# Local attention followed by two mixers on one core: score tables shared between head pairs, and two additions of the spatial product moved

## The chip, the cores and the metric

One core of a Trainium2 chip runs the whole program in one launch. The metric is device time in microseconds (us) of one execution. The kernel before was run three times; the median is 497.57 us. The engines are named as in the profile: PE (TensorE, the matrix engine), ACT (ScalarE), DVE (VectorE), POOL (GpSimd) and SP (which issues most transfers).

## What is computed

The input is an attention problem with batch 2, 8 heads, 768 positions and head size 64, all in fp32. For each head

    scores = q @ k.T / 8 + bias, with bias = -2**-(h+1) * distance
    (masked outside 8 global keys and a window of 96 keys back)
    x = softmax(scores) @ v

The slope of head h is 2^-(h+1) for h = 0 to 7. The heads' outputs are laid side by side to 512 features. Then follow two blocks: `u = x + (x mixed over positions by U V)`, `y = u + relu(u w1) w2`; and a gated block `h = relu(y w_in)`, split into u and v halves; v is normalised over features, multiplied by a 768 by 768 spatial matrix, a bias row is added, the result is multiplied by u and by `w_out`.

## The kernel before, in words

**Precision.** Most products run on PE as three passes of rounded operands: each fp32 operand is held as a rounded part (HI) and the rest (LO), and HI·HI, HI·LO and LO·HI are summed. A rounding is a copy on ACT or POOL, a rest is a subtraction on DVE or POOL.

**Attention.** The positions form 12 tiles t of 128 (six for each batch). Each tile is done in two steps of four heads, so there are 24 steps g, with t = g // 2 and hq = g % 2 the half of the heads. A step has two chunks, m = 0 and 1, and a chunk c = 2·hq + m holds two heads, 2c and 2c+1, on 64 partitions each. Each tile of 128 queries meets 256 keys (one block of 128 in the first tile of a batch); from the third tile on, the first 32 positions stand in place of the first 32 of the 256 keys, for the global keys.

- SP loads `qk_raw` (queries and keys of a tile, transposed; L372, three buffers) and `v_all` (L380). The first half of tile 0 is loaded from ACT's queue (L1126).
- `split_qk(g)` on POOL (L468 to 481): waits for the load, copies four 128x128 blocks to the HI part (a CAST of 128x512, L479) and subtracts for the LO part (a TENSOR_TENSOR of 128x512, L481). Steps 0 and 1 are split elsewhere, so that the first product starts soon: HI on ACT (L1133), LO on DVE (L719).
- `copy_k(g)` and `copy_v(g)` on POOL (L491, L501) put the 32 global positions into the key and value blocks. POOL's program, after a branch on the inputs (`windowed`, two register loads L304 and L305 and some ALU instructions), is splits 2 to 5 and then for each g: `copy_v(g)`, `copy_k(g+3)`, `split_qk(g+4)`, with some work for later stages in between (`round_V` L505 in iteration 4, `split_V` L513 in iterations 5 and 6, `split_early` L528 and `split_u` L536 from iteration 16 on).
- PE does in each loop step s: `turn(s)` (transposes of the probabilities, L1508), `turn_o(s-1)` and `turn_x(s-2)` (L1540, L1548), `scores(s+2)` (L1493), `weigh(s)` (probabilities by values, L1526). `scores(g)` waits for `qk_lo` of split g and, from the third tile of a batch on, for `copy_k(g)`; `weigh(g)` for `copy_v(g)`.
- `score_bias(g)` on DVE (L725 to 740, the instruction is at L736) adds the bias table to the scores, scales by -1/8 and takes the row's minimum in one instruction for each head. `exps(g)` on ACT (L1153) makes the exponentials.
- The tables: `bias0[:, h, :]` (128x128 for each head, for the first tile of a batch; L1136) and `bias[:, h, :]` (128x256 for each head; L1141) are copies of one distance table, scaled by the head's slope, all made on ACT. The eight of the first kind stand before ACT's branch; the eight of the second are made in pairs, between the exponentials of the first steps. `score_bias` waits in steps 0 to 3 until the table of its second head is set.

**The channel block** (about 93 to 349 us) and the products of the gated block (to 414 us) are PE work with the splits on the other engines beside it.

**The spatial product.** It is made in four groups q (two feature blocks of a batch each) as seven products of halves, each nine matmuls of 128x384 (L1826), into four banks. DVE adds them up: `add_bias(q, 0, 1)` (L1066) takes product 1 with the bias row out of bank 0, `add_bank` (L1062) takes the others, `gate_block` (L1073) multiplies by u, `split_gate` (L1080) makes the LO part after ACT has rounded the gated block (L1398). PE's third product of a group goes into bank 0 again and so waits for `add_bias(q, 0, 1)`. Every addition counts the semaphore `g_dve` up by one, seven for each group, in the same order before and after. DVE's order in a group is an order written by hand, the loop `for q in range(4)` at L1096. POOL does `add_far(q)` (L635) and splits beside it.

Of the kernel before, what the change touches and what calls it, by code (L numbers as in the profile page):

```python
# [13 lines left out]
P = 128  # L14
# [12 lines left out]
def build(nc, qk, qT, kT, v, cfg, U, V, w_ch, w_in, w_spT, b_sp, w_out, x_dram, out):  # L27
# [24 lines left out]
    with ExitStack() as ctx:  # L52
        base = (nc.sbuf_base + 63) // 64 * 64

        def at(name, shape, dtype, offset):
            return nc.alloc_sbuf_tensor_at(name, shape, dtype, offset=base + offset)
# [10 lines left out]
        part = [at(f"part{r}", [P, CT], F32, SLOT * 10 + 2048 * r) for r in range(3)]  # L67

        qk_split = at("qk_split", [P, 2, KD, 2, S], F32R, SLOT * 3)
        bias = at("bias", [P, H, KC], F32, SLOT * 9)  # L70
        bias0 = at("bias0", [P, H, P], F32, SLOT * 10)
        v_all = at("v_all", [P, NT, DM], F32, SLOT * 12 + 4096)
        prob = [at(f"prob{r}", [P, 2, KC], F32, SLOT * 14 + 2048 * r) for r in range(4)]
        probT = [at(f"probT{r}", [P, 2 * KC], F32, SLOT * 15 + 2048 * r) for r in range(4)]
# [106 lines left out]
        def sem(name):  # L181
            return ctx.enter_context(nc.semaphore(name))
# [5 lines left out]
        bias_set, iotas, ident_set, V_split = sem("bias_set"), sem("iotas"), sem("ident_set"), sem("V_split")  # L188
        qk_in = [[sem(f"qk_in{r}_{hq}") for hq in range(2)] for r in range(3)]
        v_in = [sem(f"v_in{i}") for i in range(NT)]  # L190
        qk0_hi, qk0_lo, qk_hi, qk_lo = sem("qk0_hi"), sem("qk0_lo"), sem("qk_hi"), sem("qk_lo")
        k_glob, v_glob = sem("k_glob"), sem("v_glob")
        stage_in = [sem(f"stage_in{r}") for r in range(2)]
# [23 lines left out]
            sem("wide_" + n) for n in ("qkv_in", "tables", "scored", "best", "exp")]  # L217
        w_turned, w_probT, w_out_ps, w_o, w_store, w_back, w_heads = [
            sem("wide_" + n) for n in ("turned", "probT", "out_ps", "o", "store", "back", "heads")]

        def heads(g, m):

# [229 lines left out]
        def _(pool):  # L452
# [5 lines left out]
            def count(tile, first, step, mult):  # L458
# [5 lines left out]
            pool.wait_ge(counted, 2)  # L464
            nc.gpsimd.affine_select(out=rel[:], in_=rel[:], compare_op=ALU.is_ge, fill=MASKED, base=P,
                                    pattern=[[-1, KC]], channel_multiplier=1).then_inc(iotas, 1)
            def split_qk(g):
                t, hq = divmod(g, 2)  # L468
                c, cols = slice(2 * hq, 2 * hq + 2), slice(t % NT * P, t % NT * P + P)
                hi, lo = qk_split[:, HI, c, :, cols], qk_split[:, LO, c, :, cols]  # L470
                raw = qk_raw[t % 3][:, c, :, :]
                pool.wait_ge(qk_in[t % 3][hq], 16 * (t // 3 + 1))
                if t >= NT:

                    pool.wait_ge(scored, 2 * (t - 5) + hq + 1)
                if t == NT:

                    pool.wait_ge(k_glob, globs_before(g - 1))
                nc.gpsimd.tensor_copy(hi, raw).then_inc(qk_hi, 1)  # L479
                pool.wait_ge(qk_hi, g - 1)  # L480
                nc.gpsimd.tensor_tensor(lo, raw, hi.bitcast(F32), ALU.subtract).then_inc(qk_lo, 1)  # L481
# [147 lines left out]
            def add_far(q):  # L629
# [4 lines left out]
                    pool.wait_ge(gate_lo, 4 * q)  # L634
                nc.gpsimd.tensor_tensor(gpart[3][:], gpart[0][:], b_row[:, HT:S], ALU.add).then_inc(far_bias, 1)  # L635

            near = windowed(pool)
            with pool.If(near):
                for g in range(2, 6):
# [53 lines left out]
        def _(dve):  # L693
# [28 lines left out]
            def score_bias(g, half=None):  # L722
                t = g // 2
                w = P * blocks(t)
                dve.wait_ge(scored, g + 1)  # L725
                for m in range(2) if half is None else (half,):
                    r = (2 * g + m) % 4
                    if g < 2:
                        dve.wait_ge(bias0_set, heads(g, m)[1][1] + 1)
                    elif g < 4:  # L730
                        dve.wait_ge(bias_set, heads(g, m)[1][1] + 1)
                    if g >= 2:
                        dve.wait_ge(turned, 2 * (g - 2) + m + 1)
                    for e, h in enumerate(heads(g, m)[1]):
                        k = g % 2 * 4 + 2 * m + e
                        last = vec.tensor_tensor_reduce(  # L736
                            prob[r][:, e, 0:w], s_bank[2 * (g % 2) + e][:, m * KC:m * KC + w],
                            bias0[:, h, :] if w == P else bias[:, h, :],
                            -SCALE, 3.0e38, ALU.add, ALU.min, row_min[:, k:k + 1])
                    last.then_inc(biased, 1)  # L740

            def take_probT(g):
# [351 lines left out]
                split_v_sums(q)  # L1094
            sum_v(2)
            for q in range(4):  # L1096
                add_bias(q, 0, 1)
                add_bank(q, 0, 0, 1, 2, 1)
                add_bias(q, 2, 3)

                dve.wait_ge(g_act, by_act(item_no("s", 0)))
                gate_block(q, 0, 3)
                dve.wait_ge(far_bias, q + 1)
                add_bank(q, 1, 3, 2, 4, 0)
                split_gate(q, 0)
                add_bank(q, 1, 1, 3, 5, 4)
                gate_block(q, 1, 5)
                if q == 2:

                    sum_v(3)  # L1110
                add_bank(q, 2, 0, 2, 6, 2)
                gate_block(q, 2, 6)
                split_gate(q, 1)
                add_bank(q, 3, 3, 3, 7, 0)
                gate_block(q, 3, 7)
                split_gate(q, 2)
                split_gate(q, 3)
                if q == 2:
                    split_v_ones(3)
                    split_v_sums(3)  # L1120
# [3 lines left out]
        def _(act):  # L1124
# [4 lines left out]
            sc.activation(tiny[:, 0:1], ident[:, 0:1], ACT.Exp)  # L1129
            for hq in range(2):  # L1130
                c = slice(2 * hq, 2 * hq + 2)
                act.wait_ge(qk_in[0][hq], 16)
                sc.activation(qk_split[:, HI, c, :, 0:P], qk_raw[0][:, c, :, :], ACT.Copy).then_inc(qk0_hi, 1)  # L1133
            act.wait_ge(dist0_set, 1)
            for h in range(H):
                sc.activation(bias0[:, h, :], dist0[:], ACT.Copy, scale=-(2.0 ** -(h + 1)) / SCALE  # L1136
                              ).then_inc(bias0_set, 1)

            def set_bias(first):
                for h in range(first, first + 2):  # L1140
                    sc.activation(bias[:, h, :], dist[:], ACT.Copy, scale=-(2.0 ** -(h + 1)) / SCALE  # L1141
                                  ).then_inc(bias_set, 1)

            def exps(g, half=None):
                w = P * blocks(g // 2)
# [85 lines left out]
            with act.If(near):  # L1231
                for s in range(-2, QUADS):
                    if s >= 2:
                        take_probT(s)
                    if s == 13:
                        split_stage(0)
                        copy_z(0)
                    if 0 <= s + 1 < QUADS:
                        add_eps(s + 1)
                    if s == 14:  # L1240
                        round_z(0)
                    if s in (-2, 0, 1):
                        set_bias((0, None, 4, 6)[s + 2])
                    if s >= 2:
                        take_xT(s - 2, s)
                    if 0 <= s + 2 < QUADS:
                        exps(s + 2)
                    if s == -1:
                        set_bias(2)
                    if s == 19:  # L1250
                        split_stage(1)
                    if s in (16, 18, 20, 22):
                        round_u((s - 16) // 2)
# [657 lines left out]
```

## Time and profile before

| what | value |
|---|---|
| median of 3 runs | 497.57 us (497.57 to 500.12) |
| the profiled execution: time | 497.54 us |
| the profiled execution: span from first to last instruction | 495.7 us |
| PE busy | 488.5 us, 99% |
| DVE busy | 311.8 us, 63% |
| POOL busy | 248.9 us, 50% |
| ACT busy | 222.2 us, 45% |
| moved by DMA | 36.27 MB |

The time around the span is 497.54 - 495.7 = 1.8 us. In a timeline row stand the start in us from the span's start, the length in us, the engine, the line of the kernel, the operation, what it writes and reads, the shapes and a count; several instructions of one kind in a row are merged. The square brackets hold the idle time of the engine just before it and what ended it. A name with a q behind the engine (POOLq) is the engine's instruction queue.

### The profile page before, as it was taken

How to read it: one execution, taken by the hardware profiler on the slowest of the kernel's cores; microseconds unless marked ns; L12 is line 12 of the kernel's file. 1: busy time of each engine (PE TensorE's matmuls, PEld its weight loads, DVE VectorE, ACT ScalarE, POOL GpSimd, SP SyncE). 2: the span in 40 equal slices, each digit the busy share in tenths (PEclk: the TensorE clock that was granted, in tenths of full speed). 3: DMA queues.
4: the chain of work that ended last, by engine and by line, in shares of the span. 5: the costliest groups of instructions: out<-in, count | busy, mean ns of one | idle time of the engine just before them, and what ended most of it. 6: DMA issues, size and time to landing. Idle time of an engine off the chain costs nothing.

```text
span 495.7 us, 7920 instructions
## 1 busy us (share of the span) xinstructions
PE 488.5 (99%) x2786; PEld 407.7 (82%) x2786; DVE 311.8 (63%) x726; ACT 222.2 (45%) x521; POOL 248.9 (50%) x219
## 2 busy tenths in 40 slices
PE   8999999999999999999999999999999999999997
PEld 7788677887888888888888888888888889998985
DVE  5888788511279466465655555557868888878600
ACT  7988889532234633232342322405542265333121
POOL 5898576443336666854566636323884202930000
PEclk9999999999999999999999999999999999999999
DMA  8723501132222322012222020120113000001022
GB/s 239 266 91 107 194 2 44 46 127 86 80 85 91 128 85 84 21 65 86 85 87 85 1 85 21 66 63 2 63 65 116 2 0 2 0 1 44 22 89 102
DMA packets 14552, 36.27 MB, mean 73 GB/s; under 512 B 2480, under 2 KB 2480, under 8 KB 14512
## 3 DMA queue, kind: packets, MB, share of 16 engines
q1 hardware_dynamic: 12640, 32.35, 19.5%
q10 hardware_dynamic: 1872, 3.41, 1.8%
q8 instruction: 23, 0.38, 0.3%
q14 instruction: 17, 0.14, 0.1%
HBM read 32.61 MB, written 3.15 MB: 72 GB/s over the span
## 4 chain that ended last, share of the span: by engine, by line
PE 93%; ACT 3%; DVE 2%; DMA 1%; issue 0%; SPq 0%; ACTq 0%
PE bank L1744 15%; PE bank L1470 13%; PE bank L1676 9%; PE bank L1601 9%; PE bank L1773 9%; PE bank L1766 9%; PE bank L1826 7%; PE bank L1844 7%; PE bank L1526 4%; PE bank L1508 4%; PE bank L1493 3%; ACT prob L1153 1%; PE bank L1540 1%; PE bank L1548 1%; DMA qk_raw<-in_qk 1%; DVE gated_lo L1080 1%
## 5 line engine op out<-in xcount | busy, mean ns | idle before, releaser
L520 POOL TENSOR_TENSOR w_slot<-stage,w_slot 128x1024 fp32r<-128x1024 f32 x30 | 73.3, 2451 | 64.8 <-ACT w_slot L1223 64.8
L918 DVE TENSOR_TENSOR uT<-bank,uT 128x512 f32<-128x512 f32 x68 | 45.8, 689 | 25.4 <-PE bank L1773 23.3
L1153 ACT ACTIVATE prob<-prob,row_min 128x256 f32<-128x256 f32 (+1 forms) x96 | 45.9, 480 | 7.4 <-DVE row_min L736 7.4
L1744 PE MATMUL bank<-u_op,s_slot 128*128 128x512 f32 x192 | 47.6, 389 | 0.0
L1676 PE MATMUL bank<-hid,w_slot 128*128 128x512 f32 x192 | 46.9, 393 | 0.0
L1601 PE MATMUL bank<-u_split,w_slot 128*128 128x512 f32 x192 | 46.5, 391 | 0.0
L1766 PE MATMUL bank<-hid,w_slot 128*128 128x512 f32 x192 | 46.1, 389 | 0.0
L1773 PE MATMUL bank<-hid,w_slot 128*128 128x512 f32 x192 | 46.1, 389 | 0.0
L956 DVE TENSOR_TENSOR part<-part,bank 128x512 f32<-128x512 f32 x40 | 27.4, 686 | 26.2 <-PE bank L1744 25.8
L1676 PEld LDWEIGHTS bank<-hid,w_slot 128*128 128x128 f32 x192 | 35.7, 188 | 8.2 <-issue 0.9
L1766 PEld LDWEIGHTS bank<-hid,w_slot 128*128 128x128 f32 x192 | 36.0, 188 | 7.5
L1773 PEld LDWEIGHTS bank<-hid,w_slot 128*128 128x128 f32 x192 | 36.0, 188 | 7.5
L1744 PEld LDWEIGHTS bank<-u_op,s_slot 128*128 128x128 f32 x192 | 36.0, 188 | 7.5
L1601 PEld LDWEIGHTS bank<-u_split,w_slot 128*128 128x128 f32 x192 | 35.7, 188 | 7.5 <-issue 0.2
L1223 ACT ACTIVATE w_slot<-stage 128x1024 fp32r<-128x1024 f32 x32 | 33.2, 1051 | 12.7 <-DMA stage<-in_w_ch 12.7
L736 DVE CUSTOM_DVE_ANT_0 prob<-bank,bias 128x256 f32<-128x256 f32 (+1 forms) x96 | 32.9, 398 | 7.0 <-PE bank L1493 5.5
L1744 PE MATMUL bank<-u_op,w_slot 128*128 128x512 f32 x144 | 36.5, 389 | 0.0
L928 DVE SCALAR_TENSOR_TENSOR hid<-bank,hid 128x512 fp32r<-128x512 f32 x16 | 11.1, 691 | 39.5 <-ACT hid L1276 39.3
L567 POOL TENSOR_TENSOR s_slot<-s_raw,s_slot 128x1024 fp32r<-128x1024 f32 x8 | 19.2, 2401 | 32.6 <-ACT s_slot L1228 32.6
L1844 PE MATMUL bank<-in_slot,y_split 128*128 128x512 f32 x144 | 32.8, 389 | 0.0
L1470 PE MATMUL bank<-y_split,in_slot 128*128 128x512 f32 x144 | 32.8, 389 | 0.0
L1470 PEld LDWEIGHTS bank<-y_split,in_slot 128*128 128x128 f32 x144 | 27.0, 188 | 5.6
(149 smaller groups left out, 958.7 us busy)
## 6 DMA issues: line engine op xcount, KB each, us to landing
stage<-in_w_ch SPq DMA_DIRECT2D x32, 512.0 KB, 3.3
qk_raw<-in_qk SPq DMA_DIRECT2D x23, 256.0 KB, 4.5
v_all<-in_v SPq DMA_DIRECT2D x12, 256.0 KB, 4.9
out_dram<-o_stage ACTq DMA_DIRECT2D x12, 256.0 KB, 2.0
stage<-in_w_spT SPq DMA_DIRECT2D x6, 384.0 KB, 3.1
stage<-in_w_in SPq DMA_DIRECT2D x4, 512.0 KB, 4.3
stage<-in_w_out SPq DMA_DIRECT2D x2, 512.0 KB, 3.9
V_raw<-in_V SPq DMA_DIRECT2D x4, 96.0 KB, 4.4
```

The costliest lines, as they stand in the source:

```text
L520: nc.gpsimd.tensor_tensor(dst[:, LO, :], stage[n % 2][:, 0:w], dst[:, HI, :].bitcast(F32), ALU.subtract).then_inc(w_lo, 1)
L918: vec.tensor_tensor(y, y_bank(e)[:], y, ALU.add).then_inc(y_sum, 1)
L1153: last = sc.activation(prob[r][:, e, 0:w], prob[r][:, e, 0:w], ACT.Exp, bias=row_min[:, k:k + 1], scale=-1.0, accum_out=row_sum[:, q:q + 1])
L1223: sc.activation(dst[:, HI, :], stage[n % 2][:, 0:w], ACT.Copy).then_inc(w_hi, 1)
L1470: last = mm(out_ap, lhs(a), rhs(c), start=(n == 0), stop=(n == 3 * len(terms) - 1))
L1601: last = mm(h_bank[f % 2][:], w_slot[f][:, a, k * P:(k + 1) * P], u_split[:, m, k, :], start=(k == 0 and p == 0), stop=(k == KD - 1 and p ...
L1676: last = mm(c_bank[k][:], w_slot[f][:, a, 512 + k * P:512 + (k + 1) * P], hid[f % 2][:, m, :], start=(f == 0 and a == HI and m == HI), sto ...
L1744: last = mm(seven_bank[held][:], lhs, u_op[op][:, m, k, :], start=not more and k == 0 and p == 0, stop=k == 1 and p == 2, skip_group_check ...
L1766: mm(y_bank(e + k)[:], w[r][:, a, 512 + k * P:512 + (k + 1) * P], hid2[r][n][:, m, :], start=(a == HI and m == HI), stop=False, skip_group ...
L1773: last = mm(y_bank(e + k)[:], w[r][:, a, 512 + k * P:512 + (k + 1) * P], hid2[r][n][:, m, :], start=False, stop=(a == LO), skip_group_chec ...
L1826: last = mm(s_banks(q)[held][:, 0:HT], lhs, sp_op[j][:, m, SP_AT[op], :], start=not more and j == 0 and n == 0, stop=j == TC - 1 and n == ...
L1844: last = mm(dst[:], y_split[c][:, a, k, r * P:(r + 1) * P], in_slot[k][:, m, FH:2 * FH], start=(k == 0 and p == 0), stop=(k == KD - 1 and ...
```

## The change

1. The queries of the second chunk (m = 1) of every step are multiplied by four in place before they are split: one POOL instruction `tensor_scalar` over 128x128 for each of the 24 steps (`spread_q`). For the heads of the second chunk, slope and score are both a quarter of what the first chunk's tables fit, so the scores taken four times and the first chunk's table are added, and the result is scaled by -1/32 instead of -1/8. Four tables of each kind are left (heads 0, 1, 4, 5), and ACT makes the four wide ones before the first exponentials.
2. `spread_q(0)` and `spread_q(1)` stand before POOL's branch; ACT's HI copies of tile 0 wait for them. In `split_qk` the CAST waits for the spread of its own step.
3. In the spatial product, `add_bias(1, 0, 1)` and `add_bias(2, 0, 1)` stand before `split_gate(q, 3)` of the group before them instead of behind it.

```diff
-        bias = at("bias", [P, H, KC], F32, SLOT * 9)
-        bias0 = at("bias0", [P, H, P], F32, SLOT * 10)
+        bias = at("bias", [P, 4, KC], F32, SLOT * 9)
+        bias0 = at("bias0", [P, 4, P], F32, SLOT * 10)
...
+            def spread_q(g):
+                t, hq = divmod(g, 2)
+                queries = qk_raw[t % 3][:, 2 * hq + 1, Q, :]
+                pool.wait_ge(qk_in[t % 3][hq], 16 * (t // 3 + 1))
+                nc.gpsimd.tensor_scalar(queries, queries, SPREAD, None, ALU.mult).then_inc(q_spread, 1)
+
             def split_qk(g):
...
-                pool.wait_ge(qk_in[t % 3][hq], 16 * (t // 3 + 1))
+                spread_q(g)
...
+                pool.wait_ge(q_spread, g + 1)
                 nc.gpsimd.tensor_copy(hi, raw).then_inc(qk_hi, 1)
...
+            for g in range(2):
+                spread_q(g)
             near = windowed(pool)
...
                     if g < 2:
-                        dve.wait_ge(bias0_set, heads(g, m)[1][1] + 1)
+                        dve.wait_ge(bias0_set, 2 * g + 2)
                     elif g < 4:
-                        dve.wait_ge(bias_set, heads(g, m)[1][1] + 1)
+                        dve.wait_ge(bias_set, 2 * (g - 2) + 2)
...
-                            bias0[:, h, :] if w == P else bias[:, h, :],
-                            -SCALE, 3.0e38, ALU.add, ALU.min, row_min[:, k:k + 1])
+                            (bias0 if w == P else bias)[:, 2 * (g % 2) + e, :],
+                            -SCALE / SPREAD if m else -SCALE, 3.0e38, ALU.add, ALU.min, row_min[:, k:k + 1])
...
             for q in range(4):
-                add_bias(q, 0, 1)
+                if q in (0, 3):
+                    add_bias(q, 0, 1)
...
                 split_gate(q, 2)
+                if q < 2:
+
+                    add_bias(q + 1, 0, 1)
                 split_gate(q, 3)
...
-                act.wait_ge(qk_in[0][hq], 16)
+                act.wait_ge(q_spread, hq + 1)
...
-            for h in range(H):
-                sc.activation(bias0[:, h, :], dist0[:], ACT.Copy, scale=-(2.0 ** -(h + 1)) / SCALE
-                              ).then_inc(bias0_set, 1)
...
+            for n, slope in enumerate(SLOPES):
+                sc.activation(bias0[:, n, :], dist0[:], ACT.Copy, scale=-slope / SCALE).then_inc(bias0_set, 1)
...
-                    if s in (-2, 0, 1):
-                        set_bias((0, None, 4, 6)[s + 2])
+                    if s == -2:
+                        set_bias(0)
...
-                    if s == -1:
-                        set_bias(2)
+                    if s == -2:
+                        set_bias(1)
```

## Rows read from the trace of the kernel before

**Rows 1.** The page: PE's busy time, POOL in 40 slices, the chain's shares

```profile
PE 488.5 (99%) x2786; PEld 407.7 (82%) x2786; DVE 311.8 (63%) x726; ACT 222.2 (45%) x521; POOL 248.9 (50%) x219
...
POOL 5898576443336666854566636323884202930000
...
PE 93%; ACT 3%; DVE 2%; DMA 1%; issue 0%; SPq 0%; ACTq 0%
```

**Rows 2.** Timeline of the first 22 us: ACT and DVE at the start

```profile
5.53 0.63 ACT L1133 ACTIVATE qk_split<-qk_raw 128x512 fp32r<-128x512 f32 x1 [0.55 <-DMA qk_raw<-in_qk]
...
15.21 0.71 ACT L1141 ACTIVATE bias<-dist 128x256 f32<-128x256 f32 x2
...
16.05 0.42 DVE L736 CUSTOM_DVE_ANT_0 prob<-bank,bias 128x256 f32<-128x256 f32 x1 [0.67 <-issue]
```

**Rows 3.** Timeline of PE, 9 to 50 us: scores(4), turn(3), weigh(7)

```profile
16.14 0.98 PE L1493 MATMUL bank<-qk_split 64*128 64x256 f32 x12
...
19.07 1.09 PE L1508 MATMUL bank<-ident,prob 128*128 128x128 f32 x8
...
35.28 1.09 PE L1526 MATMUL bank<-probT,v_all 128*64 128x128 f32 x16
```

**Rows 4.** Timeline of POOL, 0 to 95 us

```profile
6.29 1.14 POOL L479 CAST qk_split<-qk_raw 128x512 fp32r<-128x512 f32 x1 [3.84 <-DMA qk_raw<-in_qk]
7.51 1.28 POOL L481 TENSOR_TENSOR qk_split<-qk_raw,qk_split 128x512 fp32r<-128x512 f32 x1
...
14.48 0.53 POOL L491 CAST qk_split<-qk_split 128x128 fp32r<-128x128 f32 x2
...
17.19 0.29 POOL L491 CAST qk_split<-qk_split 128x128 fp32r<-128x128 f32 x1 [0.26 <-PE bank L1493]
...
21.58 0.29 POOL L491 CAST qk_split<-qk_split 128x128 fp32r<-128x128 f32 x1 [1.85 <-PE bank L1493]
...
24.50 0.39 POOL L501 COPY v_all<-v_all 32x256 f32<-32x256 f32 x1
25.04 0.29 POOL L491 CAST qk_split<-qk_split 128x128 fp32r<-128x128 f32 x1
...
33.86 0.39 POOL L501 COPY v_all<-v_all 32x256 f32<-32x256 f32 x1
34.20 0.28 POOL L491 CAST qk_split<-qk_split 128x128 fp32r<-128x128 f32 x1
```

**Rows 5.** Lines L304 and L638, POOL's first register load and its branch: ns min/median/max, first and last start

```profile
L304 POOLq TENSOR_LOAD <-cfg_i x1: 518/518/518, 4.0 to 4.0; - x1
...
L638 POOLq COMPARE_BRANCH  x2: 38/39/40, 5.2 to 91.1; - x2
```

**Rows 6.** POOL's groups by line and form: busy us, mean ns | idle us before

```profile
L491 POOL CAST qk_split<-qk_split 128x128 fp32r<-128x128 f32 x16 | 4.5, 288 | 9.8 <-PE bank L1493 9.6
...
L453 POOL MEMSET ident<- 128x128 f32 x1 | 0.2, 204 | 0.3 <-POOLq L1901 0.3
```

**Rows 7.** Lines L626, L479 and L1073: ns min/median/max, first and last start

```profile
L626 POOL TENSOR_TENSOR v_one<-v_far,v_one x9: 450/770/786, 423.5 to 428.7; 128x128 fp32r<-128x128 f32 x9
...
L479 POOL CAST qk_split<-qk_raw x22: 603/609/1142, 6.3 to 76.9; 128x512 fp32r<-128x512 f32 x22
...
L1073 DVE TENSOR_TENSOR gpart<-gpart,gate_u x16: 557/558/1389, 419.5 to 468.6; 128x384 f32<-128x384 f32 x16
```

**Rows 8.** Timeline of all engines, 410 to 441 us: the ends of groups 0 and 1

```profile
426.89 1.55 DVE L1080 TENSOR_TENSOR gated_lo<-gpart,gated_hi 128x384 fp32r<-128x384 f32 x2
...
428.36 0.54 DVE L1066 TENSOR_TENSOR gpart<-bank,b_row 128x384 f32<-128x384 f32 x1
428.96 1.83 PE L1826 MATMUL bank<-sp_op,v_one 128*128 128x384 f32 x9 [0.81 <-DVE gpart L1066]
...
439.66 0.56 DVE L1080 TENSOR_TENSOR gated_lo<-gpart,gated_hi 128x384 fp32r<-128x384 f32 x1
...
440.74 1.86 PE L1826 MATMUL bank<-sp_op,v_one 128*128 128x384 f32 x9 [0.59 <-DVE gpart L1066]
```

More of the change, by code:

```diff
@@ L190, in build @@
         v_in = [sem(f"v_in{i}") for i in range(NT)]
+        q_spread = sem("q_spread")
         qk0_hi, qk0_lo, qk_hi, qk_lo = sem("qk0_hi"), sem("qk0_lo"), sem("qk_hi"), sem("qk_lo")
@@ L219, in build @@
             sem("wide_" + n) for n in ("turned", "probT", "out_ps", "o", "store", "back", "heads")]
+        SPREAD = 4.0
         def heads(g, m):
@@ L1131, in _, with set_bias @@
                 c = slice(2 * hq, 2 * hq + 2)
-                act.wait_ge(qk_in[0][hq], 16)
+                act.wait_ge(q_spread, hq + 1)
                 sc.activation(qk_split[:, HI, c, :, 0:P], qk_raw[0][:, c, :, :], ACT.Copy).then_inc(qk0_hi, 1)
             act.wait_ge(dist0_set, 1)
-            for h in range(H):
-                sc.activation(bias0[:, h, :], dist0[:], ACT.Copy, scale=-(2.0 ** -(h + 1)) / SCALE
-                              ).then_inc(bias0_set, 1)
[L1139 to L1142, printed above, removed]
+            SLOPES = [2.0 ** -(h + 1) for h in (0, 1, 4, 5)]
+            for n, slope in enumerate(SLOPES):
+                sc.activation(bias0[:, n, :], dist0[:], ACT.Copy, scale=-slope / SCALE).then_inc(bias0_set, 1)
+            def set_bias(hq):
+                for n in (2 * hq, 2 * hq + 1):
+                    sc.activation(bias[:, n, :], dist[:], ACT.Copy, scale=-SLOPES[n] / SCALE).then_inc(bias_set, 1)
             def exps(g, half=None):
```

## The prediction

> **What bounds the kernel now.** I read the page first: PE is busy 99% of the span and carries 93% of the chain that ended last [rows 1]. So a cut on ACT alone is worth nothing unless it lets PE go on sooner; what counts is where PE stands still. The page's second part says where another engine is full: POOL has 8 and 9 tenths in the first slices (12.4 us each) [rows 1]. Then I read the places that the change touches.
>
> At the start, DVE's addition of a bias in the second half of its fourth step begins at 16.05 us after 0.67 us idle; the tables that it needs are made on ACT from 15.21 to 15.92 us [rows 2]. That is a real wait for a table. From 19.07 us on, where `turn(3)` starts, PE runs without a gap up to the last of the steps [rows 3]. POOL waits 1.85 us for PE before 21.58 us, so it has caught up there; then it works with hardly a gap to `copy_v(7)`, which starts at 33.86 us, ends 34.25 us [rows 4], and is needed by `weigh(7)` at 35.28 us [rows 3]. That is a margin of only 1.0 us, and all that the change adds to attention goes onto POOL. In the spatial product PE stands 0.81 and 0.59 us before the third product of groups 1 and 2, both times for DVE's L1066 [rows 8].
>
> **Tables.** Removed are four of the 128x128 copies and four of the 128x256 copies on ACT (two of the latter take 0.71 us [rows 2], so 1.4 us in all). None of it counts by itself. What counts is DVE's wait of 0.67 us at 16.05 us, which goes away: its last table is now made before the first exponentials.
>
> **The spread at the start.** ACT's second HI copy began at 5.53 us, as its data landed [rows 2]. Now one POOL instruction of 128x128 stands between. The trace has no `tensor_scalar` on POOL. The nearest rows are the CAST of 128x128 with one input, 0.29 us, the MEMSET of 128x128 with none, 0.20 us [rows 6], and the TENSOR_TENSOR of 128x128 with two inputs, 0.45 us at least and 0.77 us at the median, much of it beside DVE's work [rows 7]. I take 0.29 us, because it also reads one input. To this comes the wait for its own end: from the end of the CAST at 7.43 us to the subtraction at 7.51 us it is 0.08 us [rows 4]. So the price p of one spread in POOL's row of work is 0.37 us, with 0.28 and 0.85 us as ends. ACT's copy, and all of the first steps behind it, come 0.35 to 0.4 us later. With 0.67 us saved later, this nets a gain of at most 0.3 us at `turn(3)`, if POOL keeps up.
>
> **POOL's row of work, step by step.** Its branch comes 1.24 us after its first register load begins (4.00 to 5.24 us [rows 5]). The loads now stand behind `spread_q(1)`, which can't start before 5.53 us; so the branch ends at about 5.55 + 1.24 = 6.79 us, and `spread_q(2)` starts, with 0.16 us allowed for its way to the engine, at about 6.95 us instead of the CAST at 6.29 us [rows 4], 0.66 us later. Each split adds p. So:
> - `copy_k(4)` (the first of the two at 14.48 us [rows 4]) has splits 2 to 5 ahead of it: it ends at 14.77 + 0.66 + 4p = 16.91 us. `scores(4)` waits for it and began at 16.14 us [rows 3]: now 16.97 us. That comes back in part, as PE then stood for the probabilities (from `scores(4)` to `turn(3)` it took 2.93 us, back to back it takes 1.92 us). `turn(3)` starts at 16.97 + 1.92 = 18.89 us, 0.2 us sooner than before.
> - Up to 21.58 us POOL loses 0.66 + 6p (splits 2 to 7) less the gaps of 0.26 and 1.85 us, and less about 0.05 us of overlap that was lost there: 6p - 1.50 = 0.72 us late. Splits 8, 9 and 10 add 3p; 0.20 us are won back at 25.04 us, where the way from the copy of the values to that of the keys took 0.54 us instead of the usual 0.34 us (33.86 to 34.20) [rows 4]. `copy_v(7)` ends at 34.25 + 9p - 1.70 = 35.88 us.
> - `weigh(7)` waits for it and starts at 35.94 us instead of 35.28 us [rows 3]: attention is 9p - 2.67 = 0.66 us slower from there on. Since PE runs without a gap afterwards, nothing gives that back.
>
> Behind that, the pressure falls: splits 11 to 14 bring p each, but the two V splits are over. POOL's last copies of a batch become 3 us late, and the first load of values of the second batch waits for them; I cost that at nothing, hidden by PE's steps 10 and 11, but it is the next thing to be late. The spreads from there to the end of attention I cost at nothing too: POOL is at 5 to 8 tenths there [rows 1], and PE's own steps cover them; without that cover each would cost up to p.
>
> **The lock between POOL and DVE.** The first CAST took 1.14 us, the median one 0.61 us, and DVE's gate product took 1.39 us beside POOL and 0.56 us alone [rows 7]. The first CAST ran beside DVE's two-input subtraction, which ends at 6.96 us. If the neighbour is what made it long, the CAST now starts at 7.32 us, when the subtraction (also 0.35 us later) is over, and takes 0.61 us, while the spread before it waits up to 0.36 us for it: POOL gains about 0.25 us. I kept the 1.14 us in the sum, as the same instruction's own row, and price the other as a rival. The Trainium skill ("SBUF — State Buffer", section "SBUF: two separate sides") says that a VectorE instruction with two SBUF inputs and a GpSimd instruction that reads SBUF shut each other out for their whole length; by it the sum would be the rival's.
>
> **The spatial additions.** Two `split_gate` take 1.55 us together from 426.89 us, and `add_bias` starts at 428.36 us; behind only one of them it starts at about 427.66 us, and PE goes on 0.06 us after its end, at 428.25 instead of 428.96 us: 0.7 us [rows 8]. PE's products before it end at 428.96 - 0.81 = 428.15 us, so 0.1 us of the wait is left. At the second place the last `split_gate` starts at 439.66 us, PE at 440.74 us [rows 8]. Group 1 is 0.7 us ahead, and DVE's row there hangs on PE's products, so `add_bias` can start at 439.66 - 0.70 = 438.96 us and PE at 439.57 us: 1.17 us ahead in all. `split_gate(q, 3)`, now later by 0.54 us, holds up nothing: what is queued behind it on DVE, the second bank's addition, starts with the old order's delay at the latest, and POOL's far bias, which waits for that one, comes no later than before. From 441 us PE has no gap, so the 1.17 us stay.
>
> **Sum.** 497.54 + 0.66 - 1.17 = 497.03 us, against the profiled execution's 497.54 us, which is 0.03 us from the median. I forecast 497.0 us.
>
> **Rivals.** 0.5% is 2.49 us, about what a measurement of this kernel tells from no change.
> - *The spread is cheap* (p = 0.28 us): then `copy_v(7)` ends at 35.07 us and attention is 0.15 us faster. Time: 497.54 - 0.15 - 1.17 = 496.2 us. For it: a MEMSET of the size takes 0.20 us. Against: it reads nothing. Chance 0.25.
> - *The first CAST gets short* and the rest is as forecast: POOL's row is 0.25 us sooner, 497.03 - 0.25 = 496.8 us. For it: 1.14 against 0.61 us [rows 7]. Against: a first use of an instruction may be long by itself. Chance 0.1.
> - *The spread is dear, and the kernel slower.* POOL's `tensor_scalar` may run like its two-input form. Place: `copy_v(7)` before `weigh(7)`. Attention costs 9p - 2.67, so the kernel is slower than before from 9p = 3.84, p = 0.43 us; with 0.53 us it is 498.5 us, with 0.85 us 501.3 us. It passes 0.5% only from p = 0.70 us. Chance 0.18, a third of it above that point.
> - *The moved additions bring nothing*, because PE then waits for the next addition of the group: 497.54 + 0.66 = 498.2 us. Against: the additions behind it keep their order and start sooner. Chance 0.07.
> - The forecast's own case: 0.4.
>
> **Numbers.** The range from 495.7 to 499.6 us takes in the cheap spread with its full start gain and the dear one up to p = 0.65 us. Faster by over 0.5% would need 495.05 us, beyond every case: 0.02. Slower by over 0.5%: 0.06 for the dear spread's upper third, and 0.01 for a late load of values, so 0.07. Same: 0.91.
>
> **What would show it.** In the changed trace: 24 POOL instructions of 128x128 at about 0.29 us; `copy_v(7)` ending near 35.9 us and PE idle before `weigh(7)` for 0.8 us with POOL's L501 line as releaser; PE idle before `scores(4)` behind POOL's key copy; no DVE wait of 0.67 us at the fourth step; PE's gaps before the third product at 0.3 us or less. The forecast is wrong if POOL's spread is not near 0.29 us, if PE meets no wait for POOL at 35 us, or if attention's last PE instruction does not lie 0.4 to 0.9 us later than before.

## The result, and the profile after

| | before | after |
|---|---|---|
| median of 6 runs | 497.71 us (497.57 to 500.12) | 499.89 us (499.42 to 501.13) |
| ratio after / before | | 1.0047, 95% interval 1.0031 to 1.0062 |
| profiled execution: time, span | 497.54, 495.7 us | 501.13, 499.3 us |
| forecast | | 497.0 us, range 495.7 to 499.6 us |

The kernel became 2.2 us slower, where I forecast 0.5 us faster. That is just within the 0.5% that I had called no change, but the interval leaves out 1, and the time lies outside the range. Of several kernels here, the one before too, some executions take 1 to 3 us longer than the rest; in the two of them that were profiled (of e3 and e8 below) PE works at half its pace up to about 13 us (24 products in 2.83 us instead of 1.56 us), and they are in all medians and ratios.

The page of the kernel after answers to [rows 1]: PE is busy 2.1 us longer although it does the same work, POOL 13.7 us longer, and POOL's second to fifth slices have 9, 9, 8 and 7 tenths where they had 8, 9, 8 and 5.

```profile
PE 490.6 (98%) x2786; PEld 410.3 (82%) x2786; DVE 310.5 (62%) x726; ACT 221.0 (44%) x513; POOL 262.6 (53%) x243
...
POOL 6998789444335687635576356231886201950000
...
PE 92%; POOL 6%; issue 1%; DMA 1%; POOLq 0%; ACT 0%; ACTq 0%
```

The last line holds the first warning: POOL, which had no share in the chain that ended last, now has 6% of it. The groups by line and form name what is new. The columns are busy us and mean ns, then the idle time before:

```profile
L491 POOL CAST qk_split<-qk_raw 128x512 fp32r<-128x512 f32 x22 | 13.5, 612 | 2.4 <-POOL qk_raw L476 0.3
L476 POOL TENSOR_SCALAR qk_raw<-qk_raw 128x128 f32<-128x128 f32 x24 | 13.3, 553 | 6.5 <-DMA qk_raw<-in_qk 4.8
...
L503 POOL CAST qk_split<-qk_split 128x128 fp32r<-128x128 f32 x16 | 4.6, 289 | 1.1 <-PE bank L1511 1.1
```

The spread takes 0.55 us in the mean, the CAST of the same size 0.289 us. That CAST was my model for it.

**The start.** In the timeline of ACT and DVE, the second HI copy comes at 5.96 us instead of 5.53 us [rows 2], as forecast, and DVE's first addition of a bias at 8.22 us instead of 7.80 us:

```profile
5.96 0.63 ACT L1151 ACTIVATE qk_split<-qk_raw 128x512 fp32r<-128x512 f32 x1 [0.56 <-POOL qk_raw L476]
...
8.22 0.29 DVE L750 CUSTOM_DVE_ANT_0 prob<-bank,bias 128x128 f32<-128x128 f32 x1 [0.90 <-ACT bias L1156]
```

**POOL's row of work** (its timeline from 0 to 95 us). From 6.70 us to 54 us it has no idle time left but two waits of 0.16 us and the short ways between its own instructions; the gaps of 0.26 and 1.85 us of [rows 4] are filled.

```profile
5.37 0.56 POOL L476 TENSOR_SCALAR qk_raw<-qk_raw 128x128 f32<-128x128 f32 x1 [0.63 <-DMA qk_raw<-in_qk]
6.70 1.00 POOL L476 TENSOR_SCALAR qk_raw<-qk_raw 128x128 f32<-128x128 f32 x1 [0.78 <-DMA qk_raw<-in_qk]
7.77 0.61 POOL L491 CAST qk_split<-qk_raw 128x512 fp32r<-128x512 f32 x1
8.47 1.28 POOL L493 TENSOR_TENSOR qk_split<-qk_raw,qk_split 128x512 fp32r<-128x512 f32 x1
9.83 0.53 POOL L476 TENSOR_SCALAR qk_raw<-qk_raw 128x128 f32<-128x128 f32 x1
10.43 0.61 POOL L491 CAST qk_split<-qk_raw 128x512 fp32r<-128x512 f32 x1
...
17.67 0.53 POOL L503 CAST qk_split<-qk_split 128x128 fp32r<-128x128 f32 x2
...
38.35 0.39 POOL L513 COPY v_all<-v_all 32x256 f32<-32x256 f32 x1
```

From one CAST to the next it is 10.43 - 7.77 = 2.66 us; before it was 1.90 us (8.74 to 10.64 us). So a spread costs 0.76 us in this row: 0.53 us of work, 0.07 us from its end to the CAST that waits for it, and 0.13 us because it starts 0.08 us after the end of the subtraction ahead of it, where the CAST used to start 0.05 us before that end (the three rounded parts give 0.73). `copy_v(7)` ends at 38.74 us.

**PE** (its timeline from 5 to 46 us) waits for POOL at three places: `scores(4)`, `weigh(6)` and `weigh(7)`.

```profile
18.10 0.97 PE L1511 MATMUL bank<-qk_split 64*128 64x256 f32 x12 [0.49 <-POOL qk_split L503]
...
20.03 1.09 PE L1526 MATMUL bank<-ident,prob 128*128 128x128 f32 x8
...
33.53 1.09 PE L1544 MATMUL bank<-probT,v_all 128*64 128x128 f32 x16 [0.62 <-issue]
...
38.79 1.90 PE L1544 MATMUL bank<-probT,v_all 128*64 128x128 f32 x16 [1.80 <-POOL v_all L513]
40.62 1.91 PE L1526 MATMUL bank<-ident,prob 128*128 128x128 f32 x8
...
43.80 1.09 PE L1544 MATMUL bank<-probT,v_all 128*64 128x128 f32 x16
```

Against [rows 3], `turn(3)` is 0.96 us late and `weigh(7)` 3.51 us. Then it gets worse: `weigh(7)` and the turn behind it take 1.90 and 1.91 us, where both kinds take 1.09 us elsewhere. The windows (PE busy with its count, granted clock, DMA share, GB/s) show why:

```profile
37.00:38.00 1.00, 0.00 (x0) 1.00 0.11 25
38.00:39.00 1.00, 0.21 (x4) 0.96 0.00 0
39.00:42.00 3.00, 3.00 (x23) 0.50 0.00 0
42.00:43.00 1.00, 1.00 (x9) 0.83 0.00 0
```

Behind the wait of 1.80 us PE was granted 0.50, which is 1.2 GHz, for some 3 us. `weigh(8)` starts at 43.80 us instead of 38.73 us, 5.07 us late, so the clock added 1.56 us. PE's first product of the channel block comes 5.09 us later (98.09 against 93.00 us in the chain), and the same lateness stands at the start of the spatial product (419.19 against 414.08 us).

**The spatial product** wins back more than forecast. In the timeline, PE has no wait before the third product of groups 1 and 2 [rows 8]:

```profile
432.80 0.55 DVE L1080 TENSOR_TENSOR gpart<-bank,b_row 128x384 f32<-128x384 f32 x1
433.40 1.85 PE L1844 MATMUL bank<-sp_op,v_one 128*128 128x384 f32 x9
...
443.72 0.55 DVE L1080 TENSOR_TENSOR gpart<-bank,b_row 128x384 f32<-128x384 f32 x1
444.45 1.72 PE L1844 MATMUL bank<-sp_op,v_one 128*128 128x384 f32 x9
```

In the chain that ended last the stretch is now one piece of PE:

```profile
419.19 33.23 PE bank L1844 x189
452.42 8.20 PE bank L1488 x36
```

Before, it took 34.75 us (414.08 to 448.83 us) for these products: 1.52 us less. Together: 497.54 + 5.09 - 1.52 = 501.11 us, against 501.13 us measured. Of the six executions after, two lie at 501.1 us and four at 499.4 to 500.1 us. A sum without the clock's 1.56 us gives 497.54 + 3.51 - 1.52 = 499.53 us, which is where the four lie. That this is the difference of the groups is likely, but the mean granted clock of each execution does not show it for this kernel: it is 0.993 and 0.997 in the two, 0.996 to 1.0 in the four, and the profiled execution has a second stretch at 0.50 near its start (from 9 to 11 us), which others may have too. e6 below shows it better.

### The profile page after: what moved, and what is told of

It is laid out like the page before. It is cut to its first block, busy times and chain, and to the rows that moved or that the text cites. A ratio compares the mean times of both kernels' runs of the same rounds, so it can differ in the third digit from the quotient of the medians.

```text
span 499.3 us, 7936 instructions
## 1 busy us (share of the span) xinstructions
PE 490.6 (98%) x2786; PEld 410.3 (82%) x2786; DVE 310.5 (62%) x726; ACT 221.0 (44%) x513; POOL 262.6 (53%) x243
## 4 chain that ended last, share of the span: by engine, by line
PE 92%; POOL 6%; issue 1%; DMA 1%; POOLq 0%; ACT 0%; ACTq 0%
PE bank L1762 15%; PE bank L1488 13%; PE bank L1844 9%; PE bank L1694 9%; PE bank L1619 9%; PE bank L1791 9%; PE bank L1784 9%; PE bank L1862 7%; PE bank L1544 4%; PE bank L1526 3%; PE bank L1511 3%; POOL qk_split L493 2%; POOL qk_raw L476 1%; POOL qk_split L491 1%; PE bank L1558 1%; PE bank L1566 1%
## 5 line engine op out<-in xcount | busy, mean ns | idle before, releaser
L1862 PEld LDWEIGHTS bank<-in_slot,y_split 128*128 128x128 f32 x144 | 27.0, 188 | 5.6
```

What stands on the lines that cost most here:

```text
L1862: last = mm(dst[:], y_split[c][:, a, k, r * P:(r + 1) * P], in_slot[k][:, m, FH:2 * FH], start=(k == 0 and p == 0), stop=(k == KD - 1 and ...
```

## The experiments

The theory was: the loss is POOL's load ahead of `copy_v(7)`, at twice the price that I gave a spread, and the moved additions are a gain by themselves. The rivals were: the later start (spreads 0 and 1, POOL's later branch) is what costs; the additions bring nothing; the loss comes from the tables or DVE. In the table, "attention" is the part of the loss that is not the moved additions: the median less e1's 496.02 us, and for e2 and e6, whose additions are not moved, less the 497.6 us of the kernel before.

| kernel | median us (runs) | ratio to before, 95% interval | attention |
|---|---|---|---|
| e1, additions alone | 496.02 (12) | 0.9972 (0.9955 to 0.9989) | 0 |
| e2, all but the additions | 501.44 (6) | 1.0077 (1.0057 to 1.0097) | +3.8 |
| e3, V splits late | 497.72 (12) | 1.0003 (0.9993 to 1.0013) | +1.7 |
| e4, spreads on ACT | 496.44 (11) | 0.9974 (0.9961 to 0.9988) | +0.4 |
| e5, spread twice | 510.17 (4) | 1.0250 (1.0226 to 1.0273) | +14.2 |
| e6, POOL load alone | 499.67 (8) | 1.0040 (1.0026 to 1.0055) | +2.1 |
| e7, first tiles plain | 499.65 (11) | 1.0045 (1.0032 to 1.0058) | +3.6 |
| e8, e7 with late spreads on ACT | 496.75 (12) | 0.9984 (0.9964 to 1.0004) | +0.7 |

### The two parts of the change, each alone

e1 is the kernel before with only the two additions moved; e2 is the kernel after with them put back.

```diff
             for q in range(4):
-                add_bias(q, 0, 1)
+                if q in (0, 3):
+                    add_bias(q, 0, 1)
...
                 split_gate(q, 2)
+                if q < 2:
+                    add_bias(q + 1, 0, 1)
                 split_gate(q, 3)
```

> The kernel before with only the two moved additions. Theory A (the moved additions take PE's two gaps away, and attention pays for it): PE's waits of 0.81 and 0.59 us behind add_bias are gone, the stretch of the three first spatial groups takes 33.2 us instead of 34.75 us, and the time is 1.5 us below the kernel before (about 496.1 us). Theory B (PE's gaps closed only because attention's delay had shifted the other engines): 0 to 0.5 us below.

> The changed kernel with the two additions put back. Theory A: attention ends 4 to 5 us late as in the changed kernel and nothing is won back, so the time is 1.5 us above the changed kernel: 501.2 to 501.6 us, 3.5 to 4 us above the kernel before. Theory B: as the changed kernel, 499.5 to 500.1 us.

e1 took 496.02 us, 1.6 us less than before. In its chain, 108 matmuls follow each other without DVE between them, from 428.25 to 447.28 us; before, the same stretch had a piece of DVE's work from 435.48 to 440.74 us and ended at 448.83 us.

```profile
427.72 0.48 DVE gpart L1066
428.20 0.04 issue
428.25 19.03 PE bank L1829 x108
447.27 8.20 PE bank L1473 x36
```

e2 took 501.44 us, 1.5 us more than the whole change. So the two parts add up, and the additions are worth 1.5 us in either kernel. The rest of the change costs 3.8 us.

### Is it POOL's load, or the start?

e6 is the kernel before with a multiplication by 1.0 of the same 128x128 block in each of the 22 splits on POOL, and nothing else: the tables, the first two steps and the values stay as they were.

```diff
+                queries = qk_raw[t % 3][:, 2 * hq + 1, Q, :]
+                nc.gpsimd.tensor_scalar(queries, queries, 1.0, None, ALU.mult).then_inc(q_spread, 1)
+                pool.wait_ge(q_spread, g - 1)
                 nc.gpsimd.tensor_copy(hi, raw).then_inc(qk_hi, 1)
```

> The kernel before, with all its tables and nothing in front of POOL's branch, and one POOL multiplication by 1.0 of 128x128 in each split from step 2 on (the factor leaves the values as they are). Theory A: 9 times 0.7 us of POOL's work less the slack of 3.3 us: weigh(7) starts 2.5 to 3.5 us late, and the time is 2.5 to 4.5 us above the kernel before (500 to 502 us), with a clock drop behind PE's wait if that wait is over 1.5 us. Theory B (the start is what costs): less than 1 us above the kernel before.

e7 is the other half: the kernel after, where the first tile of each batch is not spread and has its eight tables of its own again, so that nothing stands on POOL before its branch.

```diff
+                if t % NT == 0:
+                    return
...
-            for g in range(2):
-                spread_q(g)
...
-                act.wait_ge(q_spread, hq + 1)
+                act.wait_ge(qk_in[0][hq], 16)
```

> The changed kernel with the first tile of each batch left unspread: eight 128x128 tables as before, no POOL instruction in front of the first split and of POOL's branch, and the four wide tables with POOL's spreads for the other tiles. Theory A: the backlog stays but starts 0.7 us less late, so PE's wait before weigh(7) is about 1 us instead of 1.8 us: 498.3 to 499.2 us. Theory B (the start makes the loss): the first products run as in the kernel before and the time is at or below the kernel before, 496 to 497.6 us.

e6 alone loses 2.1 us, with PE waiting for POOL at two of the three places of the kernel after (its PE timeline):

```profile
17.29 0.98 PE L1497 MATMUL bank<-qk_split 64*128 64x256 f32 x12 [1.17 <-POOL qk_split L495]
...
37.39 1.64 PE L1530 MATMUL bank<-probT,v_all 128*64 128x128 f32 x16 [1.68 <-POOL v_all L505]
38.96 1.97 PE L1512 MATMUL bank<-ident,prob 128*128 128x128 f32 x8
```

The time, 499.67 us, is a little less than I had expected (500 to 502 us): `weigh(7)` starts 2.11 us late (37.39 against 35.28 us), not 2.5 to 3.5 us. The profiled execution took 501.26 us. In it the channel block starts 3.66 us late (96.66 against 93.00 us in the chain), so 1.55 us are lost behind that wait, where the granted clock was 0.50. Six of the eight executions took 499.4 to 499.7 us at a mean granted clock of 0.999 or 1.0, and two took 501.1 and 501.3 us at 0.996. So here the two groups are the executions with and without the clock's loss.

e7 took 499.65 us, above the 498.3 to 499.2 us that I had expected, and gives back only 0.2 us of the 3.8 us. Its scores of the first two steps run at once and in full pace, and the time is lost again at the first place where PE needs POOL:

```profile
17.67 0.98 PE L1517 MATMUL bank<-qk_split 64*128 64x256 f32 x12 [1.71 <-POOL qk_split L510]
18.58 1.90 PE L1550 MATMUL bank<-probT,v_all 128*64 128x128 f32 x16
...
38.48 1.09 PE L1550 MATMUL bank<-probT,v_all 128*64 128x128 f32 x16 [0.99 <-POOL v_all L520]
```

`copy_v(7)` starts at 38.04 us, 0.31 us sooner than in the kernel after. So the later start is not what makes the loss; POOL's load is, and it alone costs 2.1 us on top of an untouched start. What the later start would cost if nothing were queued up on POOL behind it was not run by itself. The difference of e6 to the rest is in POOL's row too: there the spread starts 0.04 us before the end of the subtraction, not 0.08 us behind it, so that from CAST to CAST it is 2.55 us, a price of 0.65 us. The first CAST starts 0.48 us sooner than in the kernel after (7.29 against 7.77 us), and 8 times 0.11 us comes to it: 1.36 us; `copy_v(7)` is at 36.95 us, 1.40 us sooner. Why the same instruction overlaps in e6 and e5 and not in e7 and the kernel after stays open.

### Other work taken out of POOL's way

e3 is the kernel after with the rounding and the two splits of V, 0.83 and twice 1.8 us on POOL, moved from iterations 4 to 6 to iterations 11 and 12.

```diff
-                    if g == 4:
+                    if g == 11:
                         round_V()
-                    if g in (5, 6):
-                        split_V(g - 5, g + 3)
+                    if g in (11, 12):
+                        split_V(g - 11, g + 3)
```

> The changed kernel with round_V and the two split_V (4.5 us of POOL's work together) moved from POOL's iterations 4 to 6 to iterations 11 and 12. Theory A (POOL's backlog at copy_v(7) is what costs): POOL reaches copy_v(7) about 4.5 us sooner, PE's waits of 0.6 and 1.8 us before weigh(6) and weigh(7) and the half clock of 38.8 to 42.5 us are gone, attention ends 1 to 2 us late instead of 5 us, and the time is 496.5 to 497.5 us. Theory B (the loss is made at the start, by the later first split and the clock, and the backlog only passes it on): attention still ends over 3 us late, 499 us or more.

`copy_v(7)` stands at 33.88 us, as early as before [rows 4], and none of PE's waits is for a copy of values:

```profile
33.88 0.39 POOL L513 COPY v_all<-v_all 32x256 f32<-32x256 f32 x1
```

The time falls from 499.89 to 497.72 us, 0.2 us above the range that I had expected. So the two waits before `weigh(6)` and `weigh(7)` are worth 2.2 us of the 3.8 us; the clock's 1.56 us are not in that, as the median of the kernel after lies among its four faster executions. What is left is 1.7 us, and the kernel after shows 0.96 us of it at `turn(3)`. The other 0.7 us I can't place. e3's profiled execution took 498.51 us, not near its median: in it `turn(3)` starts 2.49 us late (21.56 us) and the channel block 2.53 us late (95.53 us), so nothing is lost between the two, but its start is not that of the median execution.

### Spreads off POOL, and a double load

e4 has all spreads on ACT, those of steps 2 to 5 between the first exponentials, the others six or five steps ahead.

```diff
+                sc.activation(queries, queries, ACT.Copy, scale=SPREAD).then_inc(q_spread, 1)
...
                     if s == -2:
+                        spread_q(3)
                         set_bias(1)
+                    if s == -1:
+                        spread_q(4)
+                        spread_q(5)
+                    if 0 <= s <= 9:
+                        spread_q(s + 6)
```

> The changed kernel with every spread as an ACT instruction (in place, scale 4) instead of a POOL one: before the HI copies for steps 0 and 1, between ACT's exponentials two to three steps ahead of their use for the others. Theory A (POOL's share is the whole loss): POOL keeps the pace of before, PE has no wait behind a copy of values, attention ends within 0.5 us of before, and with the 1.5 us of the moved additions the time is 495.7 to 496.7 us. Theory C (the spread costs wherever it stands, since the start is late by it and ACT is nearly as full there as POOL): attention ends 1 us or more late, 497 us or more.

It took 496.44 us: the loss is down to 0.4 us, with the same arithmetic and the same four tables, so the tables and DVE's part are not what cost the other 3.4 us. In the profiled execution (496.48 us) the channel block starts 0.19 us late (93.19 us), and PE waits 0.25 us for `add_bias(0, 0, 1)` before 417.68 us, a wait that neither e1 nor the kernel after has. In attention PE has one wait for POOL left, and POOL itself waits for ACT's spreads there (11 waits in attention, 5.0 us the longest):

```profile
17.18 0.98 PE L1518 MATMUL bank<-qk_split 64*128 64x256 f32 x12 [0.88 <-POOL qk_split L496]
```

e8 joins both ideas: the first tiles plain, the spreads of steps 2 and 3 on POOL, and the later ones on ACT.

```diff
-                if t % NT == 0:
+                if g not in (2, 3):
                     return
```

> As e7, with POOL's spreads for steps 2 and 3 only and ACT's for all later ones. Theory A: no wait at the start, no backlog on POOL, DVE's wait of 0.67 us for the last table gone, the two moved additions kept: 495.2 to 496.0 us, the fastest of all. Theory C (ACT's added instructions take back what its tables gave): 496.0 to 497 us.

It took 496.75 us in the median; its interval (0.9964 to 1.0004) does not set it apart from the kernel before. But that median stands between two groups: five of the twelve executions took 498.7 to 499.0 us, the profiled one among them, and seven took 495.64 to 497.14 us with 495.84 us in their middle. Ten of e1's twelve took 495.91 to 496.38 us, with 496.0 us in their middle. Which of the two is the faster is not shown, and neither is why e8 has so many of the longer ones; the times of its other executions fit Theory A.

e5 doubles the suspected cost: the spread as two multiplications by two.

```diff
-                nc.gpsimd.tensor_scalar(queries, queries, SPREAD, None, ALU.mult).then_inc(q_spread, 1)
+                nc.gpsimd.tensor_scalar(queries, queries, 2.0, None, ALU.mult).then_inc(q_spread, 1)
+                pool.wait_ge(q_spread, 2 * g + 1)
+                nc.gpsimd.tensor_scalar(queries, queries, 2.0, None, ALU.mult).then_inc(q_spread, 1)
```

> The changed kernel with each spread as two POOL multiplications by 2 instead of one by 4, which adds 0.60 us to POOL for each step. Theory A (attention's delay is nine times the price of a spread less a fixed slack): copy_v(7) and weigh(7) come 9 times 0.6 = 5.4 us later than in the changed kernel, and the time is 505 to 506 us. Theory B (one wait at the start and the clock make the loss): under 2 us above the changed kernel, 501 to 502 us.

At `copy_v(7)` the arithmetic of the prediction holds: 43.59 us, 5.24 us later than in the kernel after (POOL's timeline).

```profile
43.59 0.39 POOL L515 COPY v_all<-v_all 32x256 f32<-32x256 f32 x1
```

But the kernel is 10.3 us slower than after, where I had expected 5 to 6 us. PE waits again at copies behind `copy_v(7)`, above all in the second batch, from 77 to 97 us:

```profile
81.92 1.09 PE L1546 MATMUL bank<-probT,v_all 128*64 128x128 f32 x16 [0.45 <-POOL v_all L515]
86.98 1.09 PE L1546 MATMUL bank<-probT,v_all 128*64 128x128 f32 x16 [1.60 <-issue]
91.96 1.09 PE L1546 MATMUL bank<-probT,v_all 128*64 128x128 f32 x16 [1.10 <-POOL v_all L515]
97.03 1.09 PE L1546 MATMUL bank<-probT,v_all 128*64 128x128 f32 x16 [1.60 <-issue]
```

Summed over attention from 20 us, PE waits 2.7 us for POOL's copies and 6.1 us under "issue" just before the same products (`weigh`). `weigh(7)` starts 8.75 us later than in the kernel before (44.03 us), and the seven waits behind it add 5.60 us; the channel block starts 14.23 us late (107.23 us). Where the row says issue, the copy had ended less than the way of a signal ahead, as at 33.44 us for 33.53 us in the kernel after. So the later spreads, which I costed at nothing, were covered at the real price, and are not at twice that price.

### The price by itself

e9 is e1 with a chain of 16 instructions on POOL before its first split, over 64, 128, 256 and 512 columns: a multiplication in place, a copy, a multiplication into another tile and a two-input addition, each waiting for the one before. Its time (504.38 us, one execution) says nothing.

```diff
+            for w in (64, 128, 256, 512):
+                pool.wait_ge(probe, done)
+                nc.gpsimd.tensor_scalar(stage[0][:, 0:w], stage[0][:, 0:w], 4.0, None, ALU.mult).then_inc(probe, 1)
+                pool.wait_ge(probe, done + 1)
+                nc.gpsimd.tensor_copy(stage[1][:, 0:w], stage[0][:, 0:w]).then_inc(probe, 1)
...
```

> The kernel of the moved additions alone, with sixteen measuring instructions on POOL ahead of its first split, on buffers that are not yet in use: for 64, 128, 256 and 512 columns each a multiplication by a constant in place, a copy, the same multiplication out of place and a two-input addition. They delay the first steps, so its time says nothing. Theory 1 (the multiplication by a constant runs at the pace of the two-input form, about 2 ns a column, with a larger fixed part): near 0.53 us at 128 columns and over 1.2 us at 512. Theory 2 (it is a one-input form with the copy's pace of 0.8 ns a column and only a larger fixed part): near 0.53 us at 128 columns and 0.85 us at 512. Theory 3 (working in place is what makes it slow): out of place it takes the copy's time, about 0.2 to 0.3 us at 128 columns.

```profile
4.71 0.53 POOL L473 TENSOR_SCALAR stage<-stage 128x128 f32<-128x128 f32 x1
5.31 0.29 POOL L475 COPY stage<-stage 128x128 f32<-128x128 f32 x1
5.68 1.10 POOL L477 TENSOR_SCALAR stage<-stage 128x128 f32<-128x128 f32 x1
6.86 0.53 POOL L479 TENSOR_TENSOR stage<-stage,stage 128x128 f32<-128x128 f32 x1
...
10.63 1.49 POOL L473 TENSOR_SCALAR stage<-stage 128x512 f32<-128x512 f32 x1
12.18 0.61 POOL L475 COPY stage<-stage 128x512 f32<-128x512 f32 x1
12.87 1.49 POOL L477 TENSOR_SCALAR stage<-stage 128x512 f32<-128x512 f32 x1
14.45 1.26 POOL L479 TENSOR_TENSOR stage<-stage,stage 128x512 f32<-128x512 f32 x1
```

| columns | multiply by a constant | copy | add two tiles |
|---|---|---|---|
| 64 | 0.37 | 0.24 | 0.42 |
| 128 | 0.53 | 0.29 | 0.53 |
| 256 | 0.85 | 0.40 | 0.73 |
| 512 | 1.49 | 0.61 | 1.26 |

The table leaves out the 1.10 us of the second multiplication at 128 columns, which is taken up below. In place or not makes no difference. The multiplication by a constant costs (1.49 - 0.37) / 448 = 2.5 ns for a column, the copy (0.61 - 0.24) / 448 = 0.83 ns. The number of inputs is not what sets the price.

## Why the prediction was wrong

**The step that failed** is "the price p of one spread in POOL's row of work is 0.37 us". I took the CAST as its nearest row "because it also reads one input". Measured: 0.53 us of work and 0.2 us around it, 0.73 to 0.76 us together. The row for the other choice was in the text: the TENSOR_TENSOR of 128x128 took 0.45 us at least [rows 7], and 0.53 us in e9, just as the multiplication. The 0.2 us around the work had been taken as 0.08 us: here the inserted instruction also lost the overlap that its two neighbours had, as it did in e7, but not in e5 and e6.

**The mechanism held.** `copy_v(7)` was forecast at 34.25 + 9p - 1.70 us. With p = 0.73 us that gives 39.1 us; it ended at 38.74 us. Of the 0.4 us that are over, 0.25 us are the first spread behind the branch, at 6.70 us instead of 6.95 us. `weigh(7)` followed 0.05 us behind the copy, as priced. Attention was forecast to lose 9p - 2.67 = 0.66 us; it lost 3.51 us there. The rival "the spread is dear, and the kernel slower" named the place, the law and the point p = 0.43 us, and is what happened, at a price for which I gave a third of 0.18. As nine spreads stand before that copy, an error of 0.36 us in p became 3.2 us in the sum. That factor of nine was in my working and should have drawn the doubt to p: the sign of the result hung on one choice between two neighbouring rows, and the range should have reached 501 us.

**The start.** `copy_k(4)` was to end at 16.91 us and let `scores(4)` go at 16.97 us; it went at 18.10 us, and `turn(3)`, forecast 0.2 us sooner, came 0.96 us later. This is the same p four times over. From `scores(4)` to `turn(3)` PE took 1.93 us, as forecast (1.92 us). DVE's wait of 0.67 us for a table is indeed gone from the second half of the fourth step, and brought nothing, since by then PE stood for POOL. The copies of the table that the change saves on ACT were worth nothing by themselves, as said.

**The lock.** I kept 1.14 us for the first CAST as its own row. It took 0.61 us, and the spread ahead of it took 1.00 us where 0.53 us is the median. DVE's two-input subtraction ran beside it, from 6.62 to 7.31 us:

```profile
6.62 0.69 DVE L733 TENSOR_TENSOR qk_split<-qk_raw,qk_split 128x512 fp32r<-128x512 f32 x1 [0.39 <-ACT qk_split L1151]
```

POOL's very first spread, at 5.37 us, had taken 0.56 us. So it is the neighbour and not the first use that makes a POOL instruction long. In e9 it is the multiplication at 5.68 us, 1.10 us beside DVE's same subtraction. The Trainium skill ("SBUF — State Buffer", section "SBUF: two separate sides") says that a VectorE instruction with two SBUF inputs and a GpSimd instruction that reads SBUF shut each other out for a whole instruction. These rows agree with it. Another pair of e9 does not: POOL's multiplication at 4.71 us (0.53 us) and DVE's two-input L724 at 4.74 us (0.51 us, where it takes 0.39 us in the kernels before and after) ran side by side. In the sum it was worth little: what the CAST won the spread before it lost.

**The clock** was in no step of mine: 1.56 us behind the wait of 1.80 us, in the profiled execution and, as far as its time of 501.11 us tells, in one more of the six.

**The spatial additions** went as described, and the size was too small: 1.17 us forecast, 1.5 us measured. `add_bias` at the first place started at 432.80 - 5.11 = 427.69 us on the old time scale (forecast 427.66 us), and at the second at 438.61 us (forecast 438.96 us). I let 0.1 us of wait stand at each place from reading PE's end; e1 shows PE busy for 15.92 of 16 us and all of the next 11 us, so both waits, 0.81 and 0.59 us, are gone whole; the 0.1 to 0.2 us beyond their sum of 1.40 us I can't place. e2 and e1 show it from both sides, and the rival that the additions bring nothing is out.

**Costed at nothing, rightly:** the later spreads, up to the end of attention (no wait of PE after 46 us in the kernel after); e5 shows that this cover ends before twice the price.

## What to carry to other kernels

When a change puts a new kind of instruction into the fullest queue, find how many of them stand before the first deadline and multiply: if the sign of the sum turns between two plausible prices, the range has to hold both ends, and the price is what to measure first. On GpSimd a multiplication by a constant was priced like a two-input operation and not like a copy (0.53, 0.53 and 0.29 us for 128x128); the same spread on ScalarE, which had room, kept four tables at a loss of 0.4 us instead of 3.8 us. The lowest median of this study is that of the two additions alone, 496.02 us, which beats both the kernel before and the one after; e8 may be as good.

## What the runs showed of the hardware that I had not expected

- On POOL the multiplication of fp32 by an immediate costs 2.5 ns for a column, three times the copy's 0.83 ns, and at 512 columns it is slower (1.49 us) than the two-input addition (1.26 us). The Trainium skill ("GPSIMD Engine Reference", section "4.1 Engine selection") calls one-input operations on GpSimd roughly line-rate. That fits the copy, for which POOL took 0.29 us and VectorE 0.23 us at 128x128 in e9's trace. For the multiplication these rows speak against it, as POOL took 0.85 us for 128x256 where VectorE's `tensor_scalar` of 128x224 took 0.34 us in the same trace.
- A single wait of PE of 1.7 to 1.8 us in a stretch that is otherwise busy can be followed by half the clock. Behind waits of 1.80 us (the kernel after and e2), 1.68 us (e6), 1.71 us (e7) and 2.38 us (e5) the granted clock stood at 0.50 for about 3 us, and groups of matmuls took up to 1.9 us instead of 1.09 us. Behind 0.99 us (e7), 1.10 us and twice 1.60 us (e5) it stayed at 1.00. It does not come every time. In e6 it came in two of eight executions, by their granted clock, and they are 1.5 us longer. In e7 the granted clock does not sort the times: 0.995 and 0.996 stand in three executions of 499.2 to 499.7 us and 0.997 in all four of 500.8 to 500.9 us. In the profiled one of the three the half clock came at `weigh(2)` and `turn(3)`, ahead of the wait for POOL at `weigh(7)`; whether that wait took it up is not shown.
- In the start of the kernel after, PE was granted 0.50 from 9 to 11 us and ten products took 2.50 us instead of 1.38 us. It seems to have cost nothing there, as `scores(4)` waited for POOL anyway, and of the four faster executions the one at a granted clock of 1.0 (500.06 us) is no faster than the three at 0.996 and 0.997.
